# The first 512 tokens of the first MLP as two tiles of 256, with the head's loads and orders laid anew

## The chip, the cores and the metric

One core of one Trainium2 chip runs the whole program. The metric is the device time of one execution in microseconds (us). The core's engines work side by side, each on its own queue of instructions, and meet at semaphores: TensorE (PE) multiplies, VectorE (DVE), ScalarE (ACT) and GpSimd (POOL) do elementwise work, and SyncE (SP) and ScalarE issue DMA transfers.

## The reference

```python
for t in range(S):                                   # attention, B=4, H=8, S=768, D=48
    cur = einsum('bhd,bhe->bhde', u * kt, vt)
    y[:, :, t] = einsum('bhd,bhde->bhe', rt, state + cur)
    state = wt[..., None] * state + einsum('bhd,bhe->bhde', kt, vt)
x = y as 3072 tokens of 384
h = x @ w_in                                         # 384 -> 2048
x = (h * clip(h + 3, 0, 6) / 6) @ w_out              # 2048 -> 384
out = ((x @ w1) * (x @ w2)) @ w3 @ w_out2            # 384 -> 1024 -> 1024 -> 384
```

All inputs and the output are float32. The last two products are taken as one, with w34 = w3 @ w_out2 formed on the chip.

## The kernel before

**Attention** works on chunks of 128 tokens, two chunks to a group: 24 chunks, 12 groups. For a group the kernel builds, per head, the 128 x 128 matrix A of decayed products r.k inside each chunk, multiplies it with v and adds what the state carries. A grows in levels. Tokens up to three apart are done by elementwise products (`products_by_token` on POOL, L511; `head_products_by_token` on DVE in the head, L776) from "tokens", seven rows of 384 a token (four shifts of r, two of w, one of k, `load_tok`, L340), which DVE sums (`sum_bands`, L792) and POOL spreads into A (`start`, L528). Then there are five levels with blocks of 4, 8, 16, 32 and 64 tokens: DVE scales k and r by the decays (`scale(p, n)`, L756), TensorE multiplies (`level_products`, L1015), and a `merge` puts the result into A, on DVE for levels 0 and 1 (L815) and on ACT for 2 to 4 (L561). After them come three more steps: TURN transposes k, READ_A reads the first chunk's y and forms the new states of both, READ_B reads the second chunk's. So a group has 8 steps, (p, 0) to (p, 7). The next group's first level waits for the second state update, since both use the PSUM banks `ps_lv`. y is copied out by ACT (`y_copy`), moved across partitions by ten small DMAs on SP (`move_x`, L366), and split into a high and a low float32r half by ACT and DVE (`split_x`).

Every product of the MLPs is three float32r matmuls: high x high, low x high, high x low (L1007).

**The first MLP** runs over 6 tiles of 512 tokens and 16 pairs of `hidden(n)` and `project(n)` each, so 96 slots. hidden(n) makes 128 hidden features of the tile in `ps_h` with 9 matmuls of 512 columns; ACT clips (`clip`, L638), DVE gates (`gate`, L900), ACT and DVE split the result (`split_gated`, `rest_of_gated`), and project(n) adds its 9 matmuls into `ps_acc`. TensorE's loop over slots n does one attention step, if there is one, then project(n-1), then hidden(n+2). `step_at(slot)` (L53) says which step: number slot + LEAD with LEAD = 20, so groups 0, 1 and four levels of group 2 come ahead of the loop, and slots 0 to 75 hold the rest. ACT and DVE have the same loop, with their shares of the step behind their shares of the gating. The last tile's slots also split w1, w2 and w34 for the second MLP (`split_late`).

**The head**, ahead of the loop, is written out by hand on each engine: attention, the 8 blocks of w34 (`form_w34`, in halves of 4 matmuls; ACT stores each block, `store_w34`), and the splits of the first 9 of 16 pieces of w_in and w_out, which are loaded in turns into three staging buffers. w_in's 8 pieces come first, then w_out's. The other 7 are loaded by ACT's queue and split in slots 1, 3, 5, ... of the loop. SP issues the loads of the head in a written order, in which some wait for a buffer. w_out2 and w3T (8 blocks, in the place of w_out) come by ACT's queue. Group 1 has a matrix of its own, `A_head`, so that two groups can be in work; tokens of chunks 1 and 3 have a second buffer, `tok_b`, in the place of x.

**At the seam** to the second MLP, which has 6 tiles of 8 `product(n)` (18 matmuls of 512 columns) and `project2(n)` (12 of 384), TensorE waits for ACT's copy of the last x2 tile and then does product(0).

## Time and profile before

| | us |
|---|---|
| median of 3 runs | 1021.58 (1020.68 to 1023.0) |
| the profiled execution | 1022.78, its span 1021.0 |
| PE busy | 945.6 |
| DVE busy | 552.5 |
| ACT busy | 307.0 |
| POOL busy | 244.4 |

The trace is of one execution. A row of a timeline gives the start, the length and the operation, `out<-in`, with the shape and `xcount` where like ones are merged; in brackets stands the engine's idle time before it and what ended it. Matmuls overlap, so a length is longer than the distance to the next start. The page's slices are a 40th of the span each (25.5 us), as digits in tenths; PEclk is the granted TensorE clock, 9 standing for the higher of its two levels, 2.4 GHz.

### The profile page before, as it was taken

Reading aid. Unit: us, or ns where it says so; the run is one execution under the profiler, and the core shown is the slowest. Engines: PE = TensorE matmul, PEld = TensorE weight load, DVE = VectorE, ACT = ScalarE, POOL = GpSimd, SP = SyncE. Lnnn points to the kernel's source line nnn. Section 1 sums busy time; section 2 is a strip of 40 time slices with the busy share of each in tenths; the row PEclk is TensorE's granted clock in tenths of the full one; section 3 lists DMA queues with packets and bytes.
Section 4 is the critical chain, followed back from the end, with each engine's and each line's share of the span. In section 5 each row is a group of like instructions: output and inputs, shape, how many; then the busy total and the mean of one; then the engine's idle time right before and its main releaser. Section 6 shows DMA issues by size and latency. Waiting matters only on the chain.

```text
span 1021.0 us, 15635 instructions
## 1 busy us (share of the span) xinstructions
PE 945.6 (93%) x6320; PEld 767.9 (75%) x6320; DVE 552.5 (54%) x743; ACT 307.0 (30%) x502; POOL 244.4 (24%) x209
## 2 busy tenths in 40 slices
PE   2579849998999999999999999999999999999997
PEld 1356547777777877877787787787888888888886
DVE  1884558787877677777777853463222222222221
ACT  0113213424333333333323343453213132313222
POOL 0453335344435353535362500000000000000000
PEclk9779959999999999999999999999999999999999
DMA  9953454544342343434334101331101010100000
GB/s 281 298 165 96 131 159 118 138 112 114 110 116 84 112 132 96 133 78 151 90 109 101 55 17 31 120 114 31 63 0 62 1 62 1 62 1 31 1 31 32
DMA packets 79831, 92.84 MB, mean 91 GB/s; under 512 B 9367, under 2 KB 71822, under 8 KB 79630
## 3 DMA queue, kind: packets, MB, share of 16 engines
q1 hardware_dynamic: 69278, 82.13, 28.1%
q10 hardware_dynamic: 10480, 9.70, 3.5%
q8 instruction: 50, 0.82, 0.3%
q14 instruction: 23, 0.19, 0.1%
HBM read 76.07 MB, written 11.01 MB: 85 GB/s over the span
## 4 chain that ended last, share of the span: by engine, by line
PE 77%; DVE 11%; issue 4%; SPq 3%; ACT 2%; DMA 2%; POOL 1%; ACTq 0%; DVEq 0%
PE ps_acc L1008 9%; PE ps_lv L1036 8%; PE ps_h L1008 8%; PE ps_h L1010 8%; PE ps_h L1009 8%; PE ps_acc L1010 8%; PE ps_acc L1009 8%; PE ps_lv L1009 3%; PE ps_lv L1010 3%; PE ps_lv L1008 3%; PE ps_h L1144 3%; DVE k_sb L754 2%; DVE r_sb L754 2%; PE ps_att L1070 2%; DVE totals L754 2%
## 5 line engine op out<-in xcount | busy, mean ns | idle before, releaser
L559 ACT ACTIVATE g_hi<-gated 128x512 fp32r<-128x512 f32 x144 | 90.9, 631 | 395.6 <-DVE gated L902 262.7
L509 POOL TENSOR_TENSOR tok_a<-tok_a 128x384 f32<-128x384 f32 x120 | 144.0, 1227 | 256.0 <-DMA tok_a<-in_k 256.0
L1036 PEld LDWEIGHTS ps_lv<-r_sb,k_sb 48*128 48x128 f32 (+3 forms) x1792 | 94.4, 179 | 59.4 <-issue 46.0
L1036 PE MATMUL ps_lv<-r_sb,k_sb 48*128 48x64 f32 (+3 forms) x1792 | 101.9, 266 | 36.5 <-DVE A_own L824 23.6
L990 DVE TENSOR_TENSOR gated<-gated,ps_lv 128x512 f32<-128x512 f32 x48 | 33.1, 689 | 189.2 <-PE ps_lv L1010 189.2
L910 DVE TENSOR_TENSOR g_lo<-gated,g_hi 128x512 fp32r<-128x512 f32 x96 | 80.0, 833 | 87.5 <-ACT g_hi L559 87.5
L1008 PE MATMUL ps_acc<-g_hi,w_out_hi 128*128 128x512 f32 x288 | 122.2, 424 | 0.0
L1008 PE MATMUL ps_h<-x_hi,w_in_hi 128*128 128x512 f32 x288 | 115.5, 401 | 1.9 <-DVE gated L902 1.8
L1009 PE MATMUL ps_h<-x_hi,w_in_lo 128*128 128x512 f32 x288 | 114.7, 398 | 0.0
L1010 PE MATMUL ps_h<-x_lo,w_in_hi 128*128 128x512 f32 x288 | 114.7, 398 | 0.0
L1009 PE MATMUL ps_acc<-g_hi,w_out_lo 128*128 128x512 f32 x288 | 114.4, 397 | 0.0
L1010 PE MATMUL ps_acc<-g_lo,w_out_hi 128*128 128x512 f32 x288 | 114.3, 397 | 0.0
L642 ACT ACTIVATE gated<-ps_h,three 128x512 f32<-128x512 f32 x96 | 65.2, 680 | 43.9 <-PE ps_h L1010 43.0
L902 DVE SCALAR_TENSOR_TENSOR gated<-gated,ps_h 128x512 f32<-128x512 f32 x96 | 65.2, 679 | 12.0 <-ACT gated L642 12.0
L1008 PEld LDWEIGHTS ps_h<-x_hi,w_in_hi 128*128 128x128 f32 x288 | 54.6, 190 | 16.8 <-DVE gated L902 3.6
L1008 PEld LDWEIGHTS ps_acc<-g_hi,w_out_hi 128*128 128x128 f32 x288 | 54.3, 189 | 15.1 <-issue 1.9
L754 DVE TENSOR_TENSOR k_sb<-k_sb,totals 112x512 f32<-112x512 f32 x72 | 65.0, 903 | 0.0
L1010 PEld LDWEIGHTS ps_h<-x_lo,w_in_hi 128*128 128x128 f32 x288 | 54.7, 190 | 13.3
L1009 PEld LDWEIGHTS ps_h<-x_hi,w_in_lo 128*128 128x128 f32 x288 | 54.7, 190 | 13.0
L1010 PEld LDWEIGHTS ps_acc<-g_lo,w_out_hi 128*128 128x128 f32 x288 | 54.5, 189 | 13.1
L754 DVE TENSOR_TENSOR r_sb<-r_sb,totals 112x512 f32<-112x512 f32 x72 | 63.3, 879 | 0.0
L509 POOL TENSOR_TENSOR A_own<-corner,bmask 128x512 f32<-128x512 f32 x44 | 54.1, 1249 | 36.4 <-DVE corner L811 30.5
(96 smaller groups left out, 1574.1 us busy)
## 6 DMA issues: line engine op xcount, KB each, us to landing
tok_a<-in_r SPq DMA_DIRECT2D x85, 192.0 KB, 3.0
tok_a<-in_w SPq DMA_DIRECT2D x42, 192.0 KB, 3.7
v_sb<-in_v SPq DMA_DIRECT2D x12, 384.0 KB, 3.6
x_scratch<-x_out SPq DMA_DIRECT2D x6, 768.0 KB, 4.1
x_in<-x_scratch SPq DMA_DIRECT2D x6, 768.0 KB, 6.0
out<-x_out SPq DMA_DIRECT2D x6, 768.0 KB, 3.8
tok_a<-in_k SPq DMA_DIRECT2D x22, 192.0 KB, 4.2
w3T_sb<-in_w3T ACTq DMA_DIRECT2D x8, 512.0 KB, 19.7
```

The source lines that it names most:

```text
L509: return nc.gpsimd.tensor_tensor(dst, x, y, ALU.mult)
L559: return nc.scalar.activation(dst, src, ACT.Copy, **scale)
L642: nc.scalar.activation(gated[n % 2][:], ps_h[n % 2][:], ACT.Relu, bias=three[:]).then_inc(relu_done, 1)
L754: return nc.vector.tensor_tensor(dst, x, y, ALU.mult)
L902: nc.vector.scalar_tensor_tensor(out=gated[n % 2][:], in0=gated[n % 2][:], scalar=6.0, in1=ps_h[n % 2][:], op0=ALU.min, op1=ALU.mult).then ...
L910: nc.vector.tensor_tensor(g_lo[n % 2][:], gated[n % 2][:], g_hi[n % 2][:].bitcast(F32), ALU.subtract).then_inc(g_lo_done, 1)
L990: nc.vector.tensor_tensor(gated[n % 2][:], gated[n % 2][:], ps_lv[:, n % 2, :], ALU.mult).then_inc(ab_made, 1)
L1008: nc.tensor.matmul(psum, hi, moving_hi, start=start, stop=False)
L1009: nc.tensor.matmul(psum, lo, moving_hi, start=False, stop=False)
L1010: return nc.tensor.matmul(psum, hi, moving_lo, start=False, stop=stop)
L1036: last = nc.tensor.matmul(psum[0:count, h, first:first + C // 2] .rearrange("s (n l) -> s n l", l=size), k_g[rows, cols.start:cols.start + ...
L1144: last = nc.tensor.matmul(ps_h[f % 2][:, 0:DM], w3T_sb[f][:, kt, :], w_out2_sb[:, kt, :], start=(kt == 0), stop=(kt == NF2 - 1))
```

## The change

The first tile of 512 tokens becomes two of 256 (`WIDTHS`), so there are 7 tiles and 112 slots, of which the first 32 have matmuls and gating of 256 columns. LEAD is 10: ahead of the loop stand group 0 whole and levels 0 and 1 of group 1; slots 0 to 85 hold the other steps. `A_head` is gone. Tokens of chunk 3 use the first buffer. The pieces of w_in and w_out are taken in an order of their own (`W_ORDER`), six in the head and ten in slots 1 to 13 (`W_SPLIT`), each loaded one or two slots ahead. On SP the loads of the head have a new order, with w_out2 and w3T (now two halves) among them; the constants come by ACT's queue; tokens come in three DMAs for seven; for chunks 0 and 1 half of the moves of x are ACT's. The orders of ACT, DVE and TensorE in the head are new. Levels 0 and 1 multiply and merge 124 and 120 rows, not 128. At the seam product(0) stands before the last project, and product(1) before the wait for the x2 copy. x_hi and x_lo of the second MLP swap their buffers.

```diff
-TILES = B * S // TT
+OUT_TILES = B * S // TT
+WIDTHS = [GT, GT] + [TT] * (OUT_TILES - 1)
+TILES = len(WIDTHS)
+FIRST = [sum(WIDTHS[:t]) for t in range(TILES)]
...
+W_ORDER = [("in", 0), ("in", 1), ("in", 2), ("in", 3), ("in", 4), ("out", 0),
+           ("out", 1), ("in", 5), ("out", 2), ("out", 3), ("in", 6), ("out", 4),
+           ("out", 5), ("in", 7), ("out", 6), ("out", 7)]
+W_HEAD = 6
+W_SPLIT = {1: 6, 2: 7, 3: 8, 5: 9, 6: 10, 7: 11, 9: 12, 10: 13, 11: 14, 13: 15}
...
-LEAD = 20
+LEAD = 10
...
-        A_head = at("A_head", [P, 2, 2, PAIRS, C], F32, 0)
...
-        w3T_sb = [at(f"w3T_sb{f}", [P, NF2, P], F32, w_out_at + 4 * NF2 * P * f) for f in range(NF2)]
+        w3T_sb = [at(f"w3T_sb{i}", [P, NF2, FF2 // 2], F32, w_out_at + 2 * NF2 * FF2 * i)
+                  for i in range(2)]
...
-            return ps_acc[:, 0:2, :] if p == 0 and step != 1 else ps_lv[:]
+            if p > 0 or step == 1:
+                return ps_lv[:]
+            return ps_acc[:, 2:4, :] if step in (2, 4) else ps_acc[:, 0:2, :]
...
             def load_tok(g):
+                for n, src, on, count in ((0, r, 0, E4), (W_TOK, w, 1, 2), (K_TOK, k, 0, 1)):
+                    following = bass.AP(tokens.tensor, tokens.offset + first * DM,
+                                        [[DM, rows], [1, count * DM]])
+                    sp.dma_start(tok_at(g)[0:rows, n:n + count, :].rearrange("t n d -> t (n d)"),
+                                 following).then_inc(tok_loaded[tok_of(g)], 16)
...
-                for head in range(H):
+                for head in range(H // 2 if g < 2 else H):
...
             load_w(0)
             load_rk(0)
+            sp.dma_start(w_out2_sb[:], w_out2).then_inc(w_out2_loaded, 16)
+            load_w3T(0)
+            load_tok(1)
             load_tok(0)
-            sp.dma_start(u_sb[:], u.to_broadcast([P, DM])).then_inc(consts_loaded, 16)
-            load_tok(1)
-            for dst, src in ((lmask_in[:], level_masks[:, 0:MASKED * C // 2]),
-                             (bmask[:], block_masks), (dmask[:], diag_masks)):
-                sp.dma_start(dst, src).then_inc(consts_loaded, 16)
+            load_w3T(1)
+            load_v(0)
+            load_w_over(1)
             load_rk(1)
-            load_w_over(1)
-            for q in range(3):
-                load_weight(q)
+            load_weight(0)
+            load_weight(1)
+            load_weight(2)
             load_tok_over(2)
-            sp.wait_ge(zeroed, 1)
-            for n in (0, PR):
-                sp.dma_start(ident[n:min(n + PR, HP), n:min(n + PR, HP)],
-                             identity[0:min(PR, HP - n), 0:min(PR, HP - n)]).then_inc(ident_loaded, 16)
-            load_v(0)
+            load_weight(3)
             load_tok_over(3)
-            load_weight(3)
             load_weight(4)
             load_w_over(2)
-            load_tok_over(4)
+            load_weight(5)
             move_x(0)
             move_x(1)
             load_v_over(1)
             load_rk_over(2)
-            load_weight(5)
+            load_tok_over(4)
             load_weight(6)
-            load_w_over(3)
-            load_tok_over(5)
-            move_x(2)
-            load_tok_over(6)
-            move_x(3)
-            load_v_over(2)
-            load_rk_over(3)
             load_weight(7)
-            load_weight(8)
-            load_weight(9)
-            for p in range(2, GROUPS):
+            for p in range(1, GROUPS):
...
+                if n - 1 in W_SPLIT and W_SPLIT[n - 1] + 2 < NW:
+                    load_weight(W_SPLIT[n - 1] + 2)
+                if n in W_SPLIT:
+                    split_weight(W_SPLIT[n])
...
-                    if step == 2:
-                        pe.wait_ge(merged[0], level(0, 0))
+                if p == 0:
+                    if step > 2:
+                        pe.wait_ge(merged[0], level(0, step - 3 if step == 3 else step - 2))
                 elif step > 0:
                     pe.wait_ge(merged[p % 2], level(p, step - 1))
...
-                count = C if step < MASKED else C - size
+                count = C - size
...
+            for n in range(SLOTS):
+                if step_at(n):
+                    attention(*step_at(n))
+                if n > 0:
+                    project(n - 1)
+                if n + 2 < SLOTS:
+                    hidden(n + 2)
             pe.wait_ge(late_lo_done, LATE)
+            product(0)
+            project(SLOTS - 1)
+            product(1)
             pe.wait_ge(x2_copied, TILES)
-            product(0)
-            for n in range(1, TILES * NF2):
+            project2(0)
+            for n in range(2, OUT_TILES * NF2):
                 product(n)
                 project2(n - 1)
-            project2(TILES * NF2 - 1)
+            project2(OUT_TILES * NF2 - 1)
...
```

The new orders of the head as they are written out ((p, k) is attention(p, k)):

```
ACT   loads of u, the masks and the identity; store_w34(0), store_w34(1), split_weight(0),
      store_w34(2), merge(0, 2), store_w34(3), split_weight(1), merge(0, 3), split_weight(2),
      merge(0, 4), store_w34(4), turn_out(0), split_weight(3), y_copy(0), move_x(0),
      store_w34(5), y_copy(1), move_x(1), split_x(0), store_w34(6), split_weight(4),
      split_x(1), store_w34(7), split_weight(5), clip(0)
DVE   scale(0, 0), scale(0, 1), wait for the constants, lmask, scale(0, 2), scale(0, 3),
      scale(0, 4), head_products_by_token(0), sum_bands(0), sum_bands(1), scale(1, 0),
      merge(0, 0), merge(0, 1), split_weight(0), scale(0, 5), sum_bands(2), split_weight(1),
      scale(0, 6), scale(1, 1), split_weight(2), split_weight(3), update(0), keep(1),
      update(1), sum_bands(3), scale(1, 2), split_x(0), split_weight(4), split_x(1),
      merge(1, 0), scale(1, 3), split_weight(5), merge(1, 1)
PE    (0, 0), (0, 1), w34 0 first half, (0, 2), w34 0 second half, w34 1 to 3, (0, 3),
      w34 4 first half, (0, 4), w34 4 second half, (0, TURN), w34 5 first half, (0, READ_A),
      w34 5 second half, (0, READ_B), (1, 0), w34 6 and 7, (1, 1), hidden(0), hidden(1)
POOL  products_by_token(1), start(0), start(1), then for each group p from 1 on
      products_by_token(2p), products_by_token(2p+1), start(2p), start(2p+1)
```

## Rows read from the trace of the kernel before

**Rows 1.** The page: busy time, and two lines of its 40 slices
```profile
PE 945.6 (93%) x6320; PEld 767.9 (75%) x6320; DVE 552.5 (54%) x743; ACT 307.0 (30%) x502; POOL 244.4 (24%) x209
...
PE   2579849998999999999999999999999999999997
...
PEclk9779959999999999999999999999999999999999
```

**Rows 2.** TensorE's timeline in the head: start us, us, operation [idle before]
```profile
38.90 3.68 PE L1036 MATMUL ps_lv<-r_sb,k_sb 48*128 48x64 f32 x32 [9.87 <-DVE r_sb L754]
...
57.63 3.25 PE L1036 MATMUL ps_acc<-r_sb,k_sb 48*112 48x64 f32 x32 [7.92 <-DVE A_own L824]
...
99.92 2.85 PE L1144 MATMUL ps_h<-w_out_sb,w3T_sb 128*128 128x384 f32 x8
...
142.88 3.25 PE L1036 MATMUL ps_lv<-r_sb,k_sb 48*112 48x64 f32 x32 [7.44 <-DVE A_own L824]
...
150.61 0.79 PE L1008 MATMUL ps_h<-x_hi,w_in_hi 128*128 128x512 f32 x1
```

**Rows 3.** POOL's timeline in the head
```profile
117.18 1.96 POOL L509 TENSOR_TENSOR tok_a<-tok_a 128x384 f32<-128x384 f32 x2 [29.86 <-DMA tok_a<-in_k]
...
120.06 4.57 POOL L509 TENSOR_TENSOR tok_a<-tok_a 128x384 f32<-128x384 f32 x4
```

**Rows 4.** ACT's timeline, the clip of one slot and of the eighth after it
```profile
402.37 0.69 ACT L642 ACTIVATE gated<-ps_h,three 128x512 f32<-128x512 f32 x1 [1.37 <-PE ps_h L1010]
...
452.11 0.69 ACT L642 ACTIVATE gated<-ps_h,three 128x512 f32<-128x512 f32 x1 [1.37 <-PE ps_h L1010]
```

**Rows 5.** A loop window: length; PE, PEld, DVE, ACT, POOL busy; clock, DMA share, GB/s
```profile
402.00:452.00 50.00, 49.43 (x410) 39.48 (x408) 37.06 (x51) 16.53 (x28) 21.87 (x18) 1.00 0.36 100
```

**Rows 6.** Windows of the head, in the same columns
```profile
0.00:20.00 20.00, 0.07 (x2) 0.07 (x2) 3.58 (x7) 0.00 (x0) 0.51 (x7) 1.00 1.00 262
20.00:40.00 20.00, 10.13 (x50) 7.05 (x52) 11.60 (x11) 1.93 (x2) 8.82 (x7) 0.81 1.13 294
```

**Rows 7.** SP's timeline in the loop, the issues of one move of x
```profile
421.39 6.28 SPq L375 DMA_DIRECT2D x_sb<-y_sb  x10
```

**Rows 8.** TensorE's timeline, 18 and 12 matmuls apart without a wait
```profile
639.97 0.40 PE L1008 MATMUL ps_h<-x_hi,w_in_hi 128*128 128x512 f32 x1
...
644.17 0.40 PE L1008 MATMUL ps_h<-x_hi,w_in_hi 128*128 128x512 f32 x1
...
791.01 0.34 PE L1008 MATMUL ps_acc<-w_hi,g_hi 128*128 128x384 f32 x1
...
793.09 0.39 PE L1008 MATMUL ps_h<-x_hi,w_hi 128*128 128x512 f32 x1
```

**Rows 9.** TensorE's timeline in the loop, levels 0, 1 and 2 of a group
```profile
432.54 2.00 PE L1036 MATMUL ps_lv<-r_sb,k_sb 48*128 48x64 f32 x32
...
439.11 2.00 PE L1036 MATMUL ps_lv<-r_sb,k_sb 48*128 48x64 f32 x32 [0.18 <-DVE A_own L824]
...
445.89 1.79 PE L1036 MATMUL ps_lv<-r_sb,k_sb 48*112 48x64 f32 x32 [0.39 <-DVE A_own L824]
```

**Rows 10.** DVE's timeline in the loop
```profile
421.37 0.36 DVE L850 TENSOR_TENSOR state<-kept,ps_lv 112x192 f32<-112x192 f32 x1 [2.11 <-PE ps_lv L1092]
...
425.42 1.74 DVE L801 TENSOR_REDUCE bands<-tok_a 128x32 f32<-128x1536 f32 x1
...
429.83 0.34 DVE L850 TENSOR_TENSOR state<-kept,ps_lv 112x192 f32<-112x192 f32 x1
...
436.29 1.50 DVE L754 TENSOR_TENSOR r_sb<-r_sb,totals 112x512 f32<-112x512 f32 x1
```

**Rows 11.** TensorE's timeline at the seam
```profile
713.53 0.47 PE L1008 MATMUL ps_h<-x_hi,w_hi 128*128 128x512 f32 x1 [1.59 <-ACT x_out L559]
```

**Rows 12.** TensorE's timeline in the first tile, and the window after it
```profile
194.49 1.79 PE L1036 MATMUL ps_lv<-r_sb,k_sb 48*112 48x64 f32 x32 [2.00 <-DVE A_own L824]
...
196.00:199.00 3.00, 3.00 (x13) 2.36 (x12) 2.30 (x6) 2.59 (x6) 0.00 (x0) 0.55 0.45 131
```

More of the change, by code:

```diff
@@ L545, in _ @@
             start(1)
-            products_by_token(3)
-            start(2)
-            start(3)
-            for p in range(2, GROUPS):
+            for p in range(1, GROUPS):
                 products_by_token(2 * p)
@@ L815, in merge @@
             def merge(p, step):
+                rows = C - (E4 << step)
                 dve.wait_ge(products[p % 2], level(p, step))
```

385 lines of the change are left out of this document (172 added, 213 removed).

## The prediction

> **What bounds the kernel now.** I read the page first, then TensorE's timeline, then the timelines of the engines that release it. The page shows TensorE busy for 945.6 us of 1021.0 [rows 1], and the digits show where it isn't: almost all of the missing time lies in the first six slices (2, 5, 7, 9, 8, 4), up to 153 us. From slice 11 on every digit is 9, so there only less TensorE work could save time, and the change removes almost none: it can win in the head and lose where it thins out the loop.
>
> The head lasts until the first product of the first MLP, at 150.61 us [rows 2]. Before it TensorE does the eight blocks of w34 (8 matmuls each, 2.85 us at the full clock), two groups of attention and four levels of a third. Among its waits are 9.9 us for DVE's scaling and 7.9 and 7.4 us for DVE's merges. Behind the late ones stands POOL, which sat idle for 29.86 us until token rows of chunk 4 landed and then took 7.5 us for its seven products [rows 3]. The clock is at its lower level for parts of all this [rows 1], so the matmuls behind the waits cost about double.
>
> In the loop a slot has 18 matmuls of 512 columns and usually one attention step. Eight slots, with one whole group of attention in them, take 49.7 us [rows 4], of which TensorE is busy 49.4 and DVE 37.1 [rows 5].
>
> **Part 1: the head ends earlier.** DMA moves 262 GB/s in the first 20 us and 294 in the next [rows 6]; the change queues on SP, in this order, w and r/k of group 0 (1.4 MB), w_out2 (1.6), half of w3T (2.1), tokens 1 and 0 (1.4 each), the other half of w3T (2.1), v, w, r/k of group 1 (1.8) and three pieces of weights (1.2). At about 290 GB/s and 2.3 us of start the operands of group 0 land at 8 us, the first half of w3T at 20, tokens 0 at 30, group 1 at 43, the weights at 47. (The constants now go through ACT's queue, under 0.4 MB, beside this. DVE waits for all of them before level 1's mask; they are first in their queue and due at 12. If they came 5 us late, everything up to the tokens would shift, and the tokens, at 30, would hide it.)
> - DVE's two first scalings take until 12, level 0 runs 12 to 15, level 1 17 to 20, level 2 at 23 to 26 (each at the lower clock). The w34 blocks 0 to 3 run from 20 to about 41.
> - DVE's token products start at 30 beside POOL's, so at its slow pace for half of them, and end at 36; band sums of chunks 0 and 1 follow to 41, POOL's two starts to 44, the first merges of group 0 at 45 and 46. The same merges release level 2 at 57.6 today [rows 2], so this is 11 us sooner. Levels 3 and 4 run by 51.
> - Then a new wait. DVE's order puts the band sums of chunk 2 before the last scaling of group 0, on which the turn waits. Chunk 2's tokens go into the buffer of chunk 0, so they are asked for at 38 and come behind the queue, at 51.5; POOL's seven products end at 59, the sums at 62, the scaling at 64. TensorE stands for 12 us, and restarts at the lower clock.
> - From 64: turn, w34 block 5, the two reads and the new states until about 79; y_copy(1) at 79.5; the move of x, ten issues of 6.3 us in all on SP [rows 7], now half on SP and half on ACT's queue, so 3.1 us, and an estimated 2 for landing: 85; ACT's and DVE's halves of the split and DVE's merge of group 1 end at 89. Level 1 of group 1 runs, and the loop's first product follows at **91 us**. Behind each queued move on ACT stand a w34 copy and a weight split, all due later than the x.
>
> I take 91, with 82 if DMA or POOL run at their best rows and the clock is back at 70, and 99 if the tokens come 8 us later. The narrower level products (124 and 120 rows instead of 128) save 0.16 us a group and TensorE isn't what these chains wait for: 1 us in all. Merging on fewer partitions, the shared PSUM tensor and fewer, larger DMAs of tokens (three for seven; they save some 1.5 us of issue each) are counted at nothing beside that.
>
> **Part 2: work moves into the loop.** Six attention steps of group 1 and four of group 2 that stood ahead of the loop are now in it, one a slot.
>
> **Part 3: 32 half slots.** The first 512 tokens now take 32 slots of 256 columns. At 512 columns 18 matmuls take 4.20 us, 233 ns each; at 384 columns 12 take 2.08, 173 ns each [rows 8]. So 256 cost 113 ns along that line, 117 in proportion, and 127 if the 20 ns over 512/2.4 GHz is fixed. I take 117: 2.1 us a slot, the same sum as before; the ends are -2 and +6 us over 576 matmuls, and they vanish where TensorE waits anyway. The Trainium skill ("TensorE: Matmul & The Clock Gate", section "Back-to-back issue gap") gives N/2.4 + 2.5 ns for an isolated gap; that would be 109 ns here, but for 512 columns it gives 216 where this trace has 233, so the rows decide.
>
> TensorE's work in eight such slots is 49.4 - 16.8 = 32.6 us. The other engines don't shrink so: DVE's 37.1 us fall by 16 operations that lose 0.3 us each, to 32.3, and it waits 0.35 us a slot between its two gating steps for ACT. The steps of attention are also a chain. Level 0 starts at 432.54 and level 1 at 439.11, with TensorE idle for 0.18 just before: product, scaling, merge take 6.6 us whatever the MLP does. Level 1 to level 2 is 6.8 [rows 9], less 0.9 of gating work in it. Level 2 to 3 is TensorE's, 4.1. From level 3 to the turn DVE has a scaling, band sums, gating and a scaling, 8.1; turn to read 3.3; then from the read DVE has 8.5 us between its two state updates (421.37 to 429.83 [rows 10], with the band sums inside), less 0.6, before which level 0 of the next group may not start: 11.2 with the read itself. Sum: 6.6 + 5.9 + 4.1 + 8.1 + 3.3 + 11.2 = **39.2 us** for eight half slots. The tokens' own chain (5 us of load, 7.5 to 8.7 on POOL, 2.5 of sums, twice) is 32 and has a few us of room. The 10 weight splits that fall in slots 1 to 13, loaded one to two slots ahead by ACT's queue behind SP's tokens, add 3.8 to the first group and 2.8 to the second. So 43 + 42 + 40 + 40 = **165 us** for 32 half slots; the ends are 132 (TensorE alone) and 199 (no faster than full slots, 4 x 49.7).
>
> **Part 4: seam and small edits.** TensorE waits 1.59 us for ACT's copy of x2 before MLP 2 [rows 11]; now a product stands before that wait: 1.6 saved. One more x2 copy and store lie beside TensorE's next product. The nine late splits come in slots that hold no attention, as now, and SP's stores of x2 are asked for a slot or more before the next copy needs them.
>
> **The sum.** First product at 91; two half products 2.1; 32 half slots 165, less 1 for the first, which projects nothing, plus 2 for two full products in the last two; 54 slots with attention at 49.7/8, 335; 24 without at 4.2, 101; three half-filled ones at the seam, 6.3, less 1 for a half projection: 700.5. From MLP 2's first product to the end it is 1021.0 - 713.5 = 307.5 us. That is 1008, less 1 for the narrower products and 1.5 for what the same count gives too much on the kernel before (150.6, its first two products 9.8, 76 slots at 6.2, 18 at 4.2 and 6.3 make 713.5, where its last projection ended at 711.9): a span of **1005.5 us**. The profiled execution took 1022.78 for its span of 1021.0, and lies 1.2 above the median 1021.58: I predict **1006 us**.
>
> **Rivals.**
> A. *The half slots keep TensorE's pace.* DVE's slow scalings (r_sb 1.50 us at 436.29 [rows 10]) come with POOL at work; if they fall better, a group costs 34 to 36, the stretch 138 to 145, and the start may be at 84: 975 to 985 us. Against it is the 6.57 us chain, which is there at any pace. 0.2.
> B. *Groups stay at 49.7 us.* Place: the half slots. Mechanism: DVE's queue, in which gating, weight splits and scalings stand behind one another; each late scaling delays a level, and with it the next. Price: 199 instead of 165, 1040 us. The sum has 16 us in hand, four a group: it decides against the change from 45.3 us a group. For it: today's first tile, with the weights' splits in it, has TensorE waiting for merges at 194.49 (2.00 us [rows 12]). Against: DVE has 13 us of idle time in 50. 0.12.
> C. *The clock falls in the half slots.* After that idle stretch of 2.00 us the granted clock was 0.55 of full over the next 3 us [rows 12], and with waits of 1.6 to 2.3 us behind levels 0 and 1 of every group the new loop has many like it. At the lower level the whole stretch would be MLP work of 134 instead of 67 us and attention of up to 126 instead of 63; it would last up to 260 instead of 165: 1100. The waits absorb the first 33 us, so it decides from about four tenths of the stretch at the lower clock. 0.08. Short falls, 3 us each, I count as inside the forecast (0 to 10 us). [...]
> D. *The change gives nothing in the head*, because the w34 blocks and x moves end as late as now: the same kernel, 1015 to 1025. Against: 63 us of earlier start. 0.03.
>
> **Chances.** Forecast (990 to 1019) 0.57, A 0.2, B 0.12, C 0.08, D 0.03. The range takes in the forecast's and A's, and B's near part: 976 to 1027 us; the likeliest case alone has 990 to 1019. About 0.2% (2 us) is what can be told from no change. Faster: 0.55 + 0.2 + 0.02 (B's near end) + 0.01 = 0.78; same 0.04; slower 0.18.
>
> **What would show it.** First loop product near 91 (82 to 99); TensorE idle some 12 us before the turn of group 0, released by DVE's scaling behind band sums; 256-column matmuls 113 to 127 ns apart; eight half slots in 39 to 43 us with waits for A_own merges after levels 0 and 1; eight full slots unchanged at 49.7; no idle time at the seam. It is wrong if the loop starts after 107, if half slots take 45 us a group, or if the granted clock is low in them.

## The result and the profile after

The kernel after took 1035.11 us (median of 4 runs, 1030.11 to 1036.19) against 1022.29 (4 runs) for the one before: ratio 1.0108, interval 1.0085 to 1.0132. The forecast was 1006 us: it is 29 us off, and the kernel became slower where it was to become faster. The profiled execution took 1034.9 us, its span 1033.1.

The head did what was forecast, and more. The page of after (here and below, "answers rows 1" says that these lines stand against rows 1 of the kernel before) [answers rows 1]:

```profile
PE 964.1 (93%) x6608; PEld 804.8 (78%) x6608; DVE 554.9 (54%) x768; ACT 314.5 (30%) x535; POOL 247.6 (24%) x216
...
PE   2988687888899999999999999999999999999997
...
PEclk9998977789899999999999999999999999999999
```

There are fewer low digits at the start, and a new valley of 6, 8 and 7 in slices 5 to 11, with a lower clock under it. TensorE's timeline in the head [answers rows 2]:

```profile
16.77 3.57 PE L1023 MATMUL ps_acc<-r_sb,k_sb 48*124 48x64 f32 x32 [16.77 <-DVE r_sb L760]
...
32.02 18.33 PE L1134 MATMUL ps_h<-w_out_sb,w3T_sb 128*128 128x384 f32 x56
50.28 1.57 PE L1023 MATMUL ps_acc<-r_sb,k_sb 48*96 48x64 f32 x32
...
61.78 0.89 PE L1038 MATMUL ps_acc<-ident,k_sb 112*128 112x112 f32 x7 [2.54 <-DVE r_sb L760]
...
86.26 0.38 PE L995 MATMUL ps_h<-x_hi,w_in_hi 128*128 128x256 f32 x1
```

The first loop product comes at 86.26 us, 64 us earlier than before and 4.7 earlier than forecast. The loss is behind it, and ACT's timeline gives it with two clips, of slot 0 and of the first full slot, 32 slots later [answers rows 4]:

```profile
87.69 0.47 ACT L653 ACTIVATE gated<-ps_h,three 128x256 f32<-128x256 f32 x1 [1.02 <-PE ps_h L997]
...
278.68 0.67 ACT L653 ACTIVATE gated<-ps_h,three 128x512 f32<-128x512 f32 x1
```

The 32 half slots took 191.0 us (eights: 48.6, 52.7, 47.9, 41.9). The forecast had 165, less 1 and plus 2 for its ends: 166. From the 33rd clip to the end it is 754.4 us against 747. So -4.7, +25 and +7 make the 27.6 us between 1005.5 and 1033.1.

Windows of after, each over about eight half slots and the last over full ones [answers rows 5]:

```profile
86.00:134.00 48.00, 37.02 (x371) 34.10 (x368) 37.53 (x53) 16.38 (x32) 24.25 (x20) 0.80 0.44 139
134.00:187.00 53.00, 43.12 (x393) 39.92 (x392) 38.61 (x55) 16.06 (x33) 23.32 (x20) 0.76 0.41 123
187.00:235.00 48.00, 39.11 (x395) 36.50 (x394) 33.28 (x52) 13.69 (x29) 23.30 (x21) 0.82 0.42 119
235.00:277.00 42.00, 37.07 (x408) 33.83 (x408) 33.36 (x53) 12.68 (x28) 21.50 (x19) 0.92 0.40 116
277.00:327.00 50.00, 48.65 (x424) 39.59 (x424) 39.04 (x52) 17.54 (x31) 23.97 (x21) 1.00 0.41 120
```

In the half slots TensorE is idle for 5 to 11 us in every window, the granted clock is 0.76 to 0.92, and DVE is at work for 33 to 39 us, in the full ones for 39. The three largest of TensorE's waits from 86 to 277 us (total, times, longest):

```profile
PE ps_h L995 <- DVE gated L910: 15.2, 7, 3.7
PE ps_lv L1023 <- DVE A_own L831: 9.6, 5, 3.3
PE ps_lv L1038 <- DVE r_sb L760: 5.4, 4, 2.6
```

The first line isn't in the forecast's sum at all: the MLP's own product (hidden) waits for the gating two slots back. DVE's timeline at one such wait, and TensorE's row:

```profile
170.94 0.35 DVE L857 TENSOR_TENSOR state<-kept,ps_lv 112x192 f32<-112x192 f32 x1
171.21 0.97 DVE L760 TENSOR_TENSOR totals<-totals 112x256 f32<-112x256 f32 x1
172.10 1.48 DVE L760 TENSOR_TENSOR k_sb<-k_sb,totals 112x512 f32<-112x512 f32 x1
173.51 1.53 DVE L760 TENSOR_TENSOR r_sb<-r_sb,totals 112x512 f32<-112x512 f32 x1
174.96 1.74 DVE L807 TENSOR_REDUCE bands<-tok_a 128x32 f32<-128x1536 f32 x1
...
177.34 0.41 DVE L910 SCALAR_TENSOR_TENSOR gated<-gated,ps_h 128x256 f32<-128x256 f32 x1
```

```profile
177.81 0.58 PE L995 MATMUL ps_h<-x_hi,w_in_hi 128*128 128x256 f32 x1 [2.95 <-DVE gated L910]
...
180.03 2.33 PE L1023 MATMUL ps_lv<-r_sb,k_sb 48*124 48x64 f32 x20
```

READ_A's update, scaling and sums take the 6.4 us ahead of the gate at 177.34. In a full slot TensorE has 4.2 us of MLP matmuls to give meanwhile, here 2.1. The granted clock was 0.51 in the ten us from about the end of this wait, and 1.00 in a stretch whose only wait was 1.3 us long:

```profile
102.00:112.00 10.00, 8.68 (x111) 7.85 (x109) 6.82 (x13) 4.97 (x8) 3.21 (x3) 1.00 0.63 218
177.00:187.00 10.00, 9.19 (x58) 8.85 (x59) 6.72 (x11) 3.19 (x7) 4.76 (x5) 0.51 0.48 162
```

Last the seam, where TensorE's rows have no wait now [rows 11 had 1.59 us], and the spacing of 12 matmuls of 384 columns [answers rows 8]:

```profile
732.29 0.34 PE L995 MATMUL ps_acc<-w_hi,g_hi 128*128 128x384 f32 x1
...
801.74 0.34 PE L995 MATMUL ps_acc<-w_hi,g_hi 128*128 128x384 f32 x1
...
803.86 0.39 PE L995 MATMUL ps_h<-x_hi,w_hi 128*128 128x512 f32 x1
```

### The profile page after: what moved, and what is told of

Same layout as the page of the kernel before. It is cut to its first block, busy times and chain, and to the rows that moved or that the text cites. A ratio compares the mean times of both kernels' runs of the same rounds, so it can differ in the third digit from the quotient of the medians.

```text
span 1033.1 us, 16220 instructions
## 1 busy us (share of the span) xinstructions
PE 964.1 (93%) x6608; PEld 804.8 (78%) x6608; DVE 554.9 (54%) x768; ACT 314.5 (30%) x535; POOL 247.6 (24%) x216
## 3 DMA queue, kind: packets, MB, share of 16 engines
q1 hardware_dynamic: 56606, 86.59, 27.9%
## 4 chain that ended last, share of the span: by engine, by line
PE 76%; DVE 12%; issue 4%; DMA 4%; ACT 2%; POOL 1%; SPq 0%; ACTq 0%; DVEq 0%
PE ps_acc L995 9%; PE ps_acc L997 9%; PE ps_acc L996 8%; PE ps_lv L1023 8%; PE ps_h L995 8%; PE ps_h L997 8%; PE ps_h L996 8%; PE ps_lv L997 3%; PE ps_lv L995 3%; PE ps_lv L996 3%; DVE r_sb L760 3%; DVE k_sb L760 2%; PE ps_h L1134 2%; DVE A_own L831 2%; PE ps_acc L1057 2%
## 5 line engine op out<-in xcount | busy, mean ns | idle before, releaser
L555 ACT ACTIVATE g_hi<-gated 128x512 fp32r<-128x512 f32 (+1 forms) x160 | 94.3, 589 | 442.1 <-DVE gated L910 299.4
L995 PE MATMUL ps_h<-x_hi,w_in_hi 128*128 128x512 f32 (+1 forms) x336 | 126.8, 377 | 15.3 <-DVE gated L910 15.2
L995 PE MATMUL ps_acc<-g_hi,w_out_hi 128*128 128x512 f32 (+1 forms) x336 | 135.3, 403 | 0.0
L919 DVE TENSOR_TENSOR g_lo<-gated,g_hi 128x512 fp32r<-128x512 f32 (+1 forms) x112 | 80.3, 717 | 102.0 <-ACT g_hi L555 102.0
L1023 PEld LDWEIGHTS ps_lv<-r_sb,k_sb 48*96 48x96 f32 (+4 forms) x1792 | 99.2, 187 | 39.8 <-issue 35.5
L1023 PE MATMUL ps_lv<-r_sb,k_sb 48*96 48x64 f32 (+4 forms) x1792 | 106.8, 275 | 22.5 <-DVE A_own L831 13.2
L996 PE MATMUL ps_acc<-g_hi,w_out_lo 128*128 128x512 f32 (+1 forms) x336 | 126.2, 376 | 0.0
L997 PE MATMUL ps_acc<-g_lo,w_out_hi 128*128 128x512 f32 (+1 forms) x336 | 126.1, 375 | 0.0
L996 PE MATMUL ps_h<-x_hi,w_in_lo 128*128 128x512 f32 (+1 forms) x336 | 125.3, 373 | 0.0
L997 PE MATMUL ps_h<-x_lo,w_in_hi 128*128 128x512 f32 (+1 forms) x336 | 124.9, 372 | 0.0
L995 PEld LDWEIGHTS ps_h<-x_hi,w_in_hi 128*128 128x128 f32 x336 | 67.2, 200 | 28.1 <-DVE gated L910 13.7
L510 POOL TENSOR_TENSOR A_own<-corner,bmask 128x512 f32<-128x512 f32 x48 | 57.0, 1207 | 36.6 <-DVE corner L817 27.9
```

Source lines behind the costliest of these rows:

```text
L510: return nc.gpsimd.tensor_tensor(dst, x, y, ALU.mult)
L555: return nc.scalar.activation(dst, src, ACT.Copy, **scale)
L919: nc.vector.tensor_tensor(g_lo[n % 2][:, 0:width], gated[n % 2][:, 0:width], g_hi[n % 2][:, 0:width].bitcast(F32), ALU.subtract).then_inc( ...
L995: nc.tensor.matmul(psum, hi, moving_hi, start=start, stop=False)
L996: nc.tensor.matmul(psum, lo, moving_hi, start=False, stop=False)
L997: return nc.tensor.matmul(psum, hi, moving_lo, start=False, stop=stop)
```

## The experiments

"Half slots" is the time from clip 0 to clip 32 in a kernel's profile, with TensorE's idle time and its time at the lower clock in it. The before of each row ran on the same chip (1022.0 to 1023.7 us). The time is the median of all runs, the other three columns are of the one profiled execution, which for e7 and e9 took 3.8 and 4.6 us more than the median and for e10, e14 and e16 4.9, 3.7 and 2.5 less; so half slots of two kernels that differ by a few us aren't told apart by one profile each. In the expectations of e1 to e4, "theory T" (the clock) and "rival D" (DVE's queue) are two theories of the loss; that D isn't the prediction's rival D.

| kernel | median us (runs) | ratio to before, interval | half slots | idle | lower clock |
|---|---|---|---|---|---|
| after | 1035.11 (4) | 1.0108, 1.0085-1.0132 | 191.0 | 34.7 | 68.3 |
| e1 seam only | 1023.82 (12) | 1.0013, 0.9996-1.0029 | - | - | - |
| e2 idle matmuls, 10 | 1028.39 (5) | 1.0064, 1.0037-1.0091 | 183.3 | 20.5 | 17.1 |
| e3 spare slots | 1031.86 (4) | 1.0100, 1.0068-1.0133 | 162.0 | 27.9 | 47.8 |
| e4 sums later | 1024.89 (10) | 1.0032, 1.0005-1.0060 | 181.1 | 27.7 | 61.5 |
| e5 = e4, splits moved | 1023.55 (10) | 1.0006, 0.9989-1.0023 | 179.3 | 29.3 | 54.6 |
| e6 = e5, light POOL | 1006.54 (4) | 0.9845, 0.9812-0.9878 | 164.8 | 21.6 | 37.5 |
| e7 = e5, idle matmuls, 10 | 1023.49 (10) | 1.0016, 0.9987-1.0044 | 178.3 | 18.3 | 13.7 |
| e8 before, sums later | 1022.08 (10) | 1.0002, 0.9984-1.0020 | - | - | - |
| e9 = e5, 3 products on DVE | 1024.60 (12) | 1.0019, 0.9999-1.0039 | 185.2 | 32.5 | 58.2 |
| e10 = e6, POOL's load kept | 1014.91 (5) | 0.9924, 0.9897-0.9950 | 173.1 | 30.2 | 34.1 |
| e11 = e5, 7 products on DVE | 1020.85 (10) | 0.9976, 0.9952-1.0001 | 180.4 | 31.7 | 47.8 |
| e12 = e5, remainder later | 1021.72 (12) | 0.9983, 0.9957-1.0009 | 176.8 | 28.3 | 54.6 |
| e13 = e11, remainder later | 1020.15 (12) | 0.9971, 0.9939-1.0002 | 178.8 | 27.6 | 54.6 |
| e14 after, remainder later | 1033.76 (8) | 1.0089, 1.0062-1.0116 | 184.6 | 32.7 | 51.2 |
| e15 = e12, idle matmuls, 5 | 1021.12 (12) | 0.9966, 0.9942-0.9991 | 179.6 | 22.3 | 37.5 |
| e16 = e13, idle matmuls, 5 | 1018.32 (12) | 0.9944, 0.9921-0.9967 | 172.3 | 21.6 | 20.5 |

**e1, the seam's order alone**, put into before. The code shows TensorE's part; here and below, "..." marks lines left out, also at the ends of a cut.

```
...
             pe.wait_ge(late_lo_done, LATE)
+            product(0)
+            project(SLOTS - 1)
+            product(1)
             pe.wait_ge(x2_copied, TILES)
-            product(0)
...
```

> The kernel before, with only the seam of the change: product(0) ahead of the last project, product(1) ahead of the wait for the x2 copy. Both theories of the loss (below) say nothing of the seam. The prediction's term says 1.6 us less than before (the wait of 1.59 us goes), 1020.7 at the median. The rival: the changed kernel shows no wait at its seam and yet exactly the 315.3 us from its last clip to its end that the kernel before has, so something behind the seam became as much slower; if it comes with the seam's order, this run is at 1022 and its 384-column matmuls stand 175 to 178 ns apart instead of 172 to 175.

No change. The wait is gone, yet from the last clip to the end it is 315.29 us, and 315.30 in before. Blocks of 12 matmuls of 384 columns take 2.12 us here and in after, where rows 8 had 2.08: 48 blocks give the 1.6 back. But the order of the seam isn't what widens them. e4 and e10 have the same order and TensorE code behind the loop, and in their profiles the blocks take 2.08 and the last clip is 313.5 us from the end, 1.8 less than in before; in all other kernels with that order the blocks take 2.12. Rows of e4:

```profile
791.97 0.34 PE L995 MATMUL ps_acc<-w_hi,g_hi 128*128 128x384 f32 x1
...
794.05 0.39 PE L995 MATMUL ps_h<-x_hi,w_hi 128*128 128x512 f32 x1
```

So the order does save the wait. What makes the blocks 2.08 or 2.12 us long is open.

**e2, the clock.** Ten matmuls of 256 columns into PSUM columns nobody reads, in seven of a group's eight steps: ahead of levels 0 to 3 and the turn, and ahead of hidden in the slots of the two reads.

```
...
+                        filler(n, FILL)
                     attention(*step_at(n))
...
```

> The changed kernel, with ten idle matmuls of 256 columns (1.17 us at the full clock) put into almost every half slot where TensorE would wait: ahead of attention steps 0 to 3 and the turn, and ahead of hidden after the two reads; 1.17 us x 25, about 30 us of added TensorE work whose result nobody reads. Theory T (the clock): the 26 us that the half slots lost beyond the forecast are TensorE's lower clock after its short waits; with the waits filled the clock stays up, the 32 half slots take 165 to 178 us instead of 191, and the kernel 1008 to 1022 us in spite of 30 us more work. Rival D (DVE's queue sets the pace, the clock doesn't matter): the fillers vanish in the waits or add to them: 190 to 205 us for the stretch, 1035 to 1048 in all, with or without the clock up.

The window over e2's half slots, and that over after's:

```profile
89.19:272.48 183.29, 162.74 (x1800) 152.35 (x1800) 141.12 (x208) 58.38 (x123) 90.26 (x75) 0.95 0.43 125
```

```profile
87.69:278.68 190.99, 156.30 (x1577) 144.38 (x1576) 142.87 (x208) 58.45 (x122) 94.06 (x78) 0.82 0.42 124
```

The 230 idle matmuls are 26.9 us (117 ns each at the full clock). Without them TensorE is busy 135.8 us instead of 156.3, and its waits, the idle matmuls counted in, are 47.5 instead of 34.7. So of about 20.5 us that the lower clock had added to the matmuls, 12.8 had lain in waits that are there anyway, and 7.7 come back. That is between the two expectations (165 to 178 for the clock, 190 to 205 for DVE's queue).

**e3, seven slots without a step** in the half slots.

```
...
+    if slot in SPARE:
+        return None
+    p, k = divmod(slot + LEAD - sum(s < slot for s in SPARE), STEPS)
...
```

> The changed kernel, with seven of the 32 half slots left without an attention step (after levels 0 and 1 of groups 2 and 4, after level 0 and 1 of group 3 in part, after the first read of group 2), so attention ends seven slots later, in slot 92. The waits of the half slots are then covered by MLP work that has to be done anyway, and the full slots take over seven steps at 2 us each. Theory T: fewer waits, the clock falls in group 1 alone; stretch 130 to 145 us, 14 us more later: 990 to 1003 us. Rival D: DVE has the same work for 25 steps instead of 32 and is the limit: 191 x 25/32 = 149 and 14 more, so 1005 us. If neither the waits nor the clock move, 1035.

The half slots fell by 29 us, 4.1 for each step taken out, and what lies behind them rose by 24, 3.5 for each step, where 2 was expected; neither theory's figure was met. A half slot with its step takes 6.0 us (191.0 / 32) and a full one 6.2 (49.7 / 8): 2.1 us less of matmuls made a slot only 0.2 us shorter.

**e4, the sums of the odd token chunk behind READ_B** instead of READ_A.

```
...
                         scale(p + 1, 1)
-                    sum_bands(2 * p + 3)
                 if step == READ_B:
                     update(2 * p + 1)
+                    sum_bands(2 * p + 3)
...
```

> The changed kernel, with DVE's band sums of the second chunk moved from the first read's step to the second read's, behind the state update. In the changed kernel hidden waits four times, 3.3, 3.0, 3.7 and 2.4 us, for a gating operation that stands behind scaling and sums on DVE. Both theories take these waits for DVE's queue. Theory T: the waits shrink by the 2.4 us of the sums and with them the falls of the clock: 10 to 20 us less, 1015 to 1025. Rival D: the sums stand ahead of level 0's scaling instead, so the same work is only late elsewhere: 1030 to 1038.

10 us less, as much as the half slots lost; theory T had 10 to 20 less, rival D 1030 to 1038 us. From the start of the second read to that of the next level 0 TensorE takes 4.3 to 4.8 us instead of 7.3 to 9.3 in three groups, and 7.2 instead of 9.9 in the first. The waits of hidden for the gate fell from 15.2 to 3.8 us, those for the merges rose from 9.6 to 17.1. Of the pieces tried that cost nothing to mend, this is the largest.

**e5, no split of weights or x beside levels 0 and 1.**

```
...
-W_SPLIT = {1: 6, 2: 7, 3: 8, 5: 9, 6: 10, 7: 11, 9: 12, 10: 13, 11: 14, 13: 15}
+W_SPLIT = {1: 6, 2: 7, 3: 8, 4: 9, 5: 10, 8: 11, 9: 12, 10: 13, 11: 14, 12: 15}
...
-            if slot_of(p, k) + 2 == slot]
+            if slot_of(p, k) + 4 + (k == READ_B) == slot]
...
```

> After with the sums of the token products moved behind READ_A as before, and besides that the weight pieces split at slots 1 to 5 and 8 to 12 and the x chunks split two to three slots later, so that no split of weights or x stands in VectorE's queue in the slots of levels 0 and 1 (two weight pieces and six x chunks stood there, 1.1 and 0.72 us each on VectorE). Theory, VectorE's queue sets the pace of levels 0 and 1 (scaling and predicated merge both stand between one level's products and the next): the steps 0 to 1 and 1 to 2 of the first two half-slot groups fall from 8.1 to 8.7 us to about 7, the half slots from 181.1 to about 174 us, the time from 1025 to about 1018. Rival, the token products on GpSimd and their sums set the pace: those steps keep 8 us, 180 to 182 us for the half slots. Rival, TensorE's granted clock sets it: also 180 to 182, with half clock for some 60 us.

The sums stand behind READ_B, as in e4. It is 1.8 us less in the half slots, where 7 was expected, and no difference that the intervals resolve. On TensorE, from level 0 to 1 and 1 to 2, the first two groups' steps went from 8.1-8.7 to 6.4-7.0 us, but the third's from 6.8 and 6.7 to 8.0 and 8.6: the delay moved.

**e6, a light POOL**: e5 with three of seven products by token left out for chunks 2 to 11, so it and e10 do less work than the reference. One of the three:

```
...
+                if g >= LIGHT:
+                    times(tok[:, 2, :], tok[:, 2, :], w1_s)
...
```

> The same kernel, and for token chunks 2 to 11 (those worked on during the half slots) three of GpSimd's seven products by token are left out (the sums then take unmultiplied rows). If GpSimd's products lengthen VectorE's scalings (1.0 to 1.5 us beside them, 0.68 without) or bring the sums late, the half slots lose another 5 to 15 us (to about 160 to 168), most in levels 0 and 1. If VectorE's own queue or TensorE's clock sets the pace, they stay within 3 us of the other kernel of this pair.

**e10, the same with POOL's load kept**: three products on a spare buffer, behind the release of the sum.

```
...
+                if 4 <= g < LIGHT:
+                    for i in range(3):
...
+                        times(w34_out[:, 0, :], w34_out[:, 1, :], u_sb[:]).then_inc(kept_load, 1)
...
```

> As the light kernel (1006.5 us, half slots 164.9: three of the seven products left out for chunks 2 to 11), but for chunks 4 to 11 GpSimd runs three products of the same shape on a buffer nobody reads, after it has released the chunk's sum. So the sum may still come 3.5 us earlier, as in the light kernel, while GpSimd is as long at work beside VectorE as in the full one. Contention theory: the gain of 14 us in the half slots is mostly given back, 173 to 180 us. Chain theory (the late sums and corners held the levels): it stays at 165 to 169.

Against e5, e6 gains 17 us and e10 half of it, and the three intervals (e5, e10, e6) stand apart. DVE's scalings in the half slots, grouped (busy us, mean ns), of after, e5, e6, e10 and e11:

```profile
L760 DVE TENSOR_TENSOR r_sb<-r_sb,totals 112x512 f32<-112x512 f32 x24 | 23.7, 985 | 0.0
L760 DVE TENSOR_TENSOR k_sb<-k_sb,totals 112x512 f32<-112x512 f32 x23 | 23.1, 1003 | 0.0
```

```profile
L760 DVE TENSOR_TENSOR r_sb<-r_sb,totals 112x512 f32<-112x512 f32 x24 | 22.1, 919 | 0.0
```

```profile
L764 DVE TENSOR_TENSOR r_sb<-r_sb,totals 112x512 f32<-112x512 f32 x24 | 19.7, 821 | 0.0
L764 DVE TENSOR_TENSOR k_sb<-k_sb,totals 112x512 f32<-112x512 f32 x23 | 18.1, 789 | 0.0
```

```profile
L773 DVE TENSOR_TENSOR r_sb<-r_sb,totals 112x512 f32<-112x512 f32 x24 | 22.1, 919 | 0.0
```

```profile
L766 DVE TENSOR_TENSOR tok_a<-tok_a 128x384 f32<-128x384 f32 x48 | 23.8, 551 | 0.0
L766 DVE TENSOR_TENSOR r_sb<-r_sb,totals 112x512 f32<-112x512 f32 x24 | 16.4, 684 | 0.0
```

One scaling takes 682 ns with POOL idle and about 1500 beside it (28 and 18 of the 46 in after's half slots). e10's scalings are as long as e5's, so its load does stand for POOL's, and its 173.1 us are at the near end of what the contention theory had (173 to 180; 165 to 169 for the chain). From e10 to e6 the half slots fell by 8.2 us, all of it idle time of TensorE (30.2 to 21.6): that part goes with POOL being at work. From e5 to e10 they fell by 6.2, and the sooner sums aren't shown to be the cause: in e5's half slots DVE waited for POOL's products once, for 0.6 us. TensorE's idle time is nearly the same in both (29.3 and 30.2), its busy time fell from 150.0 to 142.8, with 34 instead of 55 us at the lower clock. Why the clock fell for less time is open, and e10's profile is a short one. The rest of e10's gain lies elsewhere: both kernels start the loop about 3 us sooner (clip 0 at 84.8 in e6 and 84.0 in e10 against 87.4), since chunks 2 and 3 are lighter in both, and e10's end has the shorter blocks of e1's text, 1.8 us.

**e7, ten idle matmuls in e5.**

> The same kernel with ten idle 256-column matmuls (about 1.2 us) ahead of seven of a group's eight steps in the half slots, which keep the clock up and add about 29 us of work. If the clock is what the half slots still lose by (about 60 us at half clock: some 25 us of matmuls running at double length), the half slots come to within 3 us of the kernel without the idle matmuls, or below it, at about 170 to 176 us. If waits on VectorE set the pace and the lower clock merely fills them, TensorE idles less and the half slots take 8 to 20 us longer.

27 us of added work changed nothing: the half slots are within 3 us of e5's, as the clock's theory allowed, but not at its 170 to 176, nor 8 to 20 us up as the other had it. The waits can hold the added work, and the clock it keeps up is worth about what it displaces.

**e8, e4's move in before.**

> The kernel before with the same one move: the sum of the odd token chunk behind READ_B instead of READ_A. Theory: at 384 columns TensorE has more to do in a slot than VectorE and hardly waits, so the move is worth nothing there, 1020 to 1023 us. Rival, the queue order costs the full slots as it does the half slots: 5 to 10 us faster.

Worth nothing there, as expected. Full slots have matmuls of 512 columns (the expectation says 384), 4.2 us of them a slot, and there the place of the sums doesn't matter.

**e9 and e11, products by token on DVE** in e5 (chunks 2 to 11; in e9 three of them, right ahead of the sum; in e11 all seven, in the loop a slot ahead of the sum). e9's:

```
...
+                    times(tok[:, 2, :], tok[:, 2, :], tok[:, W_TOK, :])
+                    times(tok[:, 0, :], tok[:, 0, :], tok[:, K_TOK, :])
+                    times(tok[:, 3, :], tok[:, 3, :], tok[:, W_TOK + 1, :]).then_inc(tok_products, 1)
...
```

> The kernel with sums later and splits moved (1023.6 us, 179.3 us for the half slots), and for token chunks 2 to 11 the three products by token that the light kernel left out are made by VectorE right ahead of the chunk's sum: nothing is left out. In the trace VectorE's 112x512 scalings take 683 ns alone and 1463 to 1494 beside GpSimd, GpSimd's products 1.1 to 1.2 us. Theory, GpSimd beside VectorE makes the half slots slow: eight chunks there take 3.5 us off GpSimd each and cost VectorE about 1.6; the half slots fall from 179.3 to 168 to 175 and the time to 1012 to 1020. Rival, VectorE's busy time alone decides: 13 us more of it, the half slots at 185 to 192, the time at 1030 or more.

> As the kernel with sums later and splits moved, but for token chunks 2 to 11 VectorE makes all seven products by token (about 0.53 us each by the 683 ns of a 512-wide scaling alone, 3.7 us a chunk), one slot ahead of the chunk's sum, and GpSimd none; GpSimd keeps the two starts of A. Contention theory: VectorE's scalings and remainders run at their undisturbed length, but 7.4 us a group are added to a queue that was 36 of 43 us busy; the half slots come to 165 to 180, the time to 1010 to 1024, about even with three products on VectorE. If the beside-GpSimd length is not the cause, VectorE's queue becomes the bound at 44 us a group or more and the half slots take 190 or more.

e9 gained nothing: the scalings won back 3 us, the products took 13, and the half slots are at 185.2, the figure of the rival (DVE's busy time), though the time isn't at its 1030. In e11 the scalings run undisturbed (684 ns above) and DVE is busy for 142.0 us, as in e5 (141.7) with the products on POOL: in the half slots POOL's help with them is worth nothing to DVE. The time is 0.3% lower, not resolved.

**e12, e13, e14, the gated tile's remainder behind scaling and merge**, in e5, e11 and after.

```
...
+                if first:
+                    levels_of(*first)
                 rest_of_gated(n)
...
```

> The kernel with sums later and splits moved (1023.6 us, half slots 179.3), and in the 20 half slots that carry a level step VectorE makes the step's scaling and merge before the remainder of the gated tile. In the traces so far the remainder stands ahead of them and waits 0.48 us for ScalarE's copy, then takes 0.43 to 0.66, so the next level's product gets its merge 0.9 us late; and a half slot's matmuls give only about 2.1 us of cover between two levels. Theory, the round trip from level product over VectorE to the next level product is the bound of the level steps: 20 times 0.5 to 0.9 us less, half slots at 162 to 170, the time at 1007 to 1014. Rival, the bound is the total of VectorE's busy time beside GpSimd: 0.48 us of idle goes elsewhere, 176 to 180, the time stays at 1021 to 1024. Rival, the later remainder now holds the projection: 182 or more.

> The same order in the kernel whose seven token products for chunks 2 to 11 are on VectorE (1020.9 us, half slots 180.4 in its profile). If the round trip is the bound, 160 to 172 us for the half slots and 1003 to 1012 for the time, the best of all; if VectorE's total is, it gains 5 us at most.

> After with this order alone, sums and splits where the change has them (1035.1 us, half slots 191.0). Round trip: 8 to 16 us less, 1019 to 1027. If waits behind READ_A's sums and late token chunks bound it instead: 1031 to 1035.

Misses for the theory that the round trip between TensorE and DVE bounds the level steps: 0.7 to 1.8 us, none resolved, where it had 8 to 18. In the half slots e12 has 2.5 us less, e13 1.6 and e14 6.4. All three times lie where the rivals had them. DVE's timeline in e12, and TensorE's rows of levels 1 and 2:

```profile
177.99 0.29 DVE L762 TENSOR_TENSOR totals<-totals 112x128 f32<-112x128 f32 x1 [2.16 <-PE ps_lv L1032]
178.20 0.68 DVE L762 TENSOR_TENSOR k_sb<-k_sb,totals 112x512 f32<-112x512 f32 x1
178.81 0.68 DVE L762 TENSOR_TENSOR r_sb<-r_sb,totals 112x512 f32<-112x512 f32 x1
179.41 1.24 DVE L833 COPY_PREDICATED A_own<-lmask,ps_lv 124x1024 f32<-124x1024 uint8 x1
...
182.79 0.35 DVE L762 TENSOR_TENSOR totals<-totals 112x64 f32<-112x64 f32 x1 [1.51 <-PE ps_lv L1032]
```

```profile
180.79 1.90 PE L1032 MATMUL ps_lv<-r_sb,k_sb 48*120 48x64 f32 x32 [0.60 <-DVE A_own L833]
...
187.31 2.04 PE L1032 MATMUL ps_lv<-r_sb,k_sb 48*112 48x64 f32 x28 [2.31 <-DVE A_own L833]
```

DVE now waits for TensorE's level product (2.16 and 1.51 us) and TensorE for DVE's merge (0.60 and 2.31), in turn. From 88 to 275 us DVE waited in e5 16.2 us for ACT's copy of the gated tile and 8.4 for level products; in e12 it is 6.5 and 20.4, so most of what the order freed on DVE became another wait. Levels 0 to 2 did get shorter, by 2.2 us a group over three groups, and 5.1 us of these 6.6 were lost again at the reads of one group, where DVE waits 2.2 us for ACT's half of a weight split (ACT had waited 1.4 for the piece's DMA) and then has the split and three scalings beside POOL ahead of the gate, for which hidden waits 4.1 us. All this is from one profile of each.

**e15, e16, five idle matmuls** instead of ten, in e12 and e13.

> The kernel with sums later, splits moved and the remainder behind scaling and merge (1021.7 us; half slots 176.8, TensorE idle 28.3 us and 55 us of them at half clock), with five idle 256-column matmuls (0.6 us) ahead of seven of a group's eight steps in the half slots, 14 us of work in waits that are 28 us long. If the lower clock lengthens the part of the round trip that TensorE has (level products 3.2 to 3.6 us instead of 1.9), half clock falls to under 30 us and the half slots to 165 to 172, the time to 1010 to 1017. If VectorE's part alone sets the trip, 176 to 184 us.

> The same five idle matmuls in the kernel whose token products are on VectorE too (1020.2 us, half slots 178.8). Clock in the round trip: 165 to 173 us for the half slots, the time 1007 to 1015. VectorE alone: 178 to 186 us, the time 1020 to 1027.

e15 doesn't differ from e12 (half slots 179.6 us), as it should if DVE's part alone set the trip. e16 is at 1018.32 us, 0.56% under before, the best of all that do the whole work; it and e15 are the two whose intervals lie clear below before. Its half slots are where the clock's theory had them (165 to 173), its time isn't (1007 to 1015). The window over its half slots:

```profile
85.86:258.20 172.34, 150.75 (x1678) 139.99 (x1677) 143.25 (x263) 57.66 (x122) 19.14 (x17) 0.94 0.45 132
```

Beside after (above) POOL's busy time is 19 instead of 94 us and the clock 0.94 instead of 0.82. Its interval overlaps e13's, so what the five matmuls add to it stays open.

## Why the prediction was wrong

- **The head, 91 us**: right, 86.3. Within it two times were off and made up for each other: group 0's operands landed at 13 instead of 8 (DVE stood idle for 12.3 us at the start), and the wait of 12 us ahead of the turn was 2.54. POOL's timeline [answers rows 3] has chunk 2's products at 49.39 instead of 51.5, and TensorE, whose levels 3 and 4 began at 50.28 and 55.31 instead of being over at 51, came to the turn at 59.2 instead of 52. Why the operands came 5 us late is open. The clock stayed up until 91 us. POOL's rows:

```profile
49.39 2.00 POOL L510 TENSOR_TENSOR tok_a<-tok_a 128x384 f32<-128x384 f32 x2 [3.71 <-DMA tok_a<-in_k]
...
52.31 4.75 POOL L510 TENSOR_TENSOR tok_a<-tok_a 128x384 f32<-128x384 f32 x4
```

- **256 columns, 117 ns**: right at the full clock, 116 to 117; 213 at the lower.
- **"43 + 42 + 40 + 40 = 165 us for 32 half slots"**: this is the step that failed, by 25 us. Its chain for one group (39.2 us) was built of the full slots' segments and missed three things. For three groups the six segments measured 7.7, 6.9, 6.3, 8.8, 3.6 and 13.8 us on average, where it had 6.6, 5.9, 4.1, 8.1, 3.3 and 11.2. (1) It let only the attention steps wait. At READ_A it had DVE's 8.5 us between the state updates, but not that the gate for the next hidden product queues behind them: 15.2 us of waits, and moving the sums made the half slots 10 us shorter (e4). (2) It left the lower clock out of the 165, as "Short falls, 3 us each", worth 0 to 10 us: eight falls, 68 us in all, cost 8, as far as idle matmuls give it back (e2). (3) It took DVE's and POOL's operations as they fall in full slots, where TensorE covers them. The work beside POOL was worth 8 us (e10 to e6). The other 6 between e5's 179 and e6's 165 went with less time at the lower clock, the cause of which is open; that e6 meets the forecast is chance, as it does less work. The pieces overlap and don't add up to 25: e6 and e10 leave work out, and what one edit frees the next wait partly takes.
- **The chain's mechanism** was right in kind, that a step takes about 6 us whatever the MLP does (6.0 in a half slot, 6.2 in a full one). That the DVE-TensorE round trip sets levels 0 and 1 is only partly shown: in e12 each waits for the other, but a shorter trip brought 2.5 us in the half slots where 9 to 17 was expected. I have no run that tells which wait ends last in every step.
- **Rival B** (groups stay at 49.7 us, DVE's queue, 1040 us) is what happened, at 47.8 us a group and 1035; it had 0.12. Its own decision point, 45.3 us a group, was right. I held 13 us of DVE idle time in 50 against it. That was the error: idle time of an engine with a strict order says nothing of its latency. DVE is idle for 48 of 191 us in the half slots and still is what TensorE waits for; 18 of the 48 are its own waits for ACT's copy of the gated tile, 16 those for TensorE's level product, 10 those for ACT's halves of the weight splits.
- **Rival C**, the clock: the falls came, 36% of the stretch, just under the four tenths from which it was to decide, and at 6.8 or 10.2 us each, not 3. Its price of up to 95 us was for the whole stretch at the lower clock, which no run has; at 36% the cost was 8 us, as most of the slow matmuls lay in waits, which is as it said. Of the eight falls in the half slots seven came with a wait of 2.4 to 3.7 us and one with 1.4.
- **The seam, -1.6 us**: the wait went as forecast, and e4 and e10 show the gain (1.8 us), but after and e1 don't: there the 384-column matmuls, 3.6 ns wider apart, gave it back. Why they are stays open. It and the 1 us for narrower products are part of the 7 us behind the 33rd clip; I have not split the rest. Full slots, 49.7 for eight: right (47.5 to 52.3, mean 49.2 over six).

Still open: what the last 6 us of e16's half slots over the forecast (172.3 to 166) are made of, and how much of e16's gain is the clock's. Untested is whether weight pieces that land sooner would help; e5 moved splits and loads together.

## What to carry to other kernels

When a tile is halved, only the matmuls halve. The gate fell from 680 to 410 ns, and an attention step's operations stayed as long as they were. The in-order queue of the engine that serves them keeps its operations, and every burst in it that the long tile used to cover (here 6.4 us of scaling and sums ahead of a gate) can become a wait; look for the longest run between two operations that TensorE needs, not for the engine's busy share. A lower clock need not cost what its share of the time suggests (68 us of it cost 8 here): measure it by filling the waits before you pay for a fix. And before work is given to an idle engine, see what it does to the one beside it: GpSimd's products cost VectorE as much time as making them itself (e11).

## What the runs showed of the hardware

- VectorE's operations with two SBUF inputs get longer beside GpSimd: 112x512 scalings from 682 to 1500 ns, the remainder of 512 columns from 692 to 1146 on average (761 to 1500). Not each one does: of the 13 remainders of 256 columns that lie wholly beside GpSimd's work in after, 8 took 425 to 427 ns, as alone. With one input in PSUM (the gate, 680 ns alone and 674 beside) or one input (the sum, 1743 and 1749) they don't get longer. The Trainium skill ("SBUF — State Buffer", section "SBUF: two separate sides") says that GpSimd and a VectorE operation with two SBUF inputs share a pair of ports that one of them holds for a whole instruction. The traces agree in these four kinds of operation. That doesn't explain all of e6's gain, as e10 gave back only half.
- A VectorE product of 128x384 takes 551 ns (e11), GpSimd's 1.0 us alone and 1.2 in the loop. A scaling beside it costs VectorE 0.8 us more; so e11 could move 56 products of the half slots to VectorE without adding to its busy time.
- Eight falls of the granted clock to half, with waits of 1.4 to 3.7 us at or shortly before their start, make 68 us in after's half slots (waits of 1.3 us at 105.7 and 1.8 us at 114.5 passed without one); with 26.9 us of idle matmuls in the waits (e2) it is 17 us.
- The same 12 float32r matmuls of 384 columns take 2.08 us in the profiles of before, e4, e8 and e10 and 2.12 in all the others, constant within each profile (e1); with 48 blocks that is 1.8 us.
